# Issuing the zero fill of y_rows from Pool in three parts during the attention, in a fused attention, expert and MLP kernel

## The chip, the cores and the metric

The kernel runs on one core of a Trainium2 chip. The metric is device time in microseconds (us) of one launch, taken over repeated executions; lower is better. The core has a matrix engine (PE), a vector engine (DVE), a scalar engine (ACT), a general engine (Pool, also called GpSimd) and a sync engine (SP) that does little but issue DMAs. Engines run side by side, each through its own list of instructions in order, and meet at semaphores. Data moves between HBM and on-chip SBUF on 16 DMA engines. A DMA that SP issues goes into one hardware queue ("q1 hardware_dynamic" in the profile), one that Pool issues into a software queue ("q0 software_dynamic"); both are served by the same 16 engines.

## The reference

Three stages run one after the other. Attention: 4 batches, 8 heads, 576 positions, head size 64; four heads see a causal band of 32 positions, the other four see every 32nd position. Its output is x, 2304 token rows of 512. Experts: a token whose skip score is above zero goes to the one of 8 experts that its gate picks; its row becomes x plus a gated expert output, all others keep x. MLP: 512 to 2048, leaky ReLU, back to 512.

```python
x = np.ascontiguousarray(attn_out.transpose(0, 2, 1, 3)).reshape(B * S, H * D)
# experts
do_compute = x @ w_skip > 0
xc = x[do_compute]
e_idx = np.argmax(xc @ w_gate, axis=1)
for e in range(E):
    mask = e_idx == e
    h = np.maximum(xc[mask] @ w1[e], 0.0)
    y[mask] = gate_w[mask, None] * (h @ w2[e])
out[do_compute] = xc + y
# MLP
h = x @ w_in
return np.maximum(0.01 * h, h) @ w_out
```

## The kernel before

**Attention.** Each batch has 11 groups of queries (`NG`): 6 of the local heads, 5 of the strided ones. PE transposes q and k in 16 chunks per batch, computes scores, transposes the probabilities and multiplies by v; ACT copies chunks and takes exponentials; DVE subtracts maxima and normalises into `xo`. A loop runs over batches 0 to 2 with the next batch's chunks woven in, and the last batch follows. SP feeds it by hand-written order (`batch`, L449): after each group's `xo` it stores rows to the HBM tensor `x_rows` (`x_store`, L386), loads v of the next batch (`v_load`: L396 for a local group, four DMAs on L401 for a strided one) and, at groups 2, 4, 6 and 8, half of q or k of the batch after that into `q_st` and `k_st` (L409). These staging tiles are copied into `q_in` and `k_in` by three engines. Pool has three of these copies in each of its three loop turns (L616 to L624), in the order q half 0, k half 0, k half 1; each waits for PE to be done with the old chunks and for the load. ACT does q half 1 (L842).

**Routing.** When a batch's `x_rows` have landed, SP loads them back token by token (`x_load`, L441 to L447). PE computes the gate scores, DVE turns them by a long chain of small steps into a list of token numbers per tile of 160 rows (`tok_idx`), and Pool gathers the rows of tile 0 in two halves (`gather_x(0)`, L667), which PE transposes (L1480) before the first expert matmul (L1497).

**Experts.** Tiles 0 to 21 at most; 7 are certain to hold rows written in any case. SP keeps the weights of the next tile coming in a ring of 8 pieces (`half_load`, L360) and stores each tile's result to the HBM tensor `y_rows` (L493, L495). While tiles run, Pool gathers the next tile's rows, loads and splits the MLP weights (`stage_load`, L684), and sorts.

**MLP.** Pool gathers x and y rows in sorted order (L744), PE does the two matmuls in six steps, and results are scattered out. It takes the last 415 us, PE nearly always busy.

**The zero fill.** The gather of `y_rows` in the MLP also reads rows that no tile has written: slots past an expert's last token, and the one row `SKIP` (3520) for tokens that are passed on. Rows 1120 to 3519, `(E - 1) * TILE` to `SKIP`, and row 3520 are therefore set to zero from `zrow`, a tile of zeros in SBUF that Pool sets in its set-up (L596). SP issues both DMAs once, after the last `x_load` and ring pieces 4 to 7 of tile 0 (L480, L481). The big one moves 2400 rows of 2 KB: `zrow` has `FILL` = 120 partitions, each written out `ZC` = 20 times. SP waits for both (L520) before its first tile step, since from then on tiles may store into the same rows, and again at its end (L550); Pool waits for them (L766) before the MLP's first gathers.

Of the kernel before, what the change touches and what calls it, by code (L numbers as in the profile page):

```python
# [17 lines left out]
TILE = 160  # L18
# [4 lines left out]
def attention_experts_mlp(nc, q, k, v, w_skip, w_gate, w1, w2, w_in, w_out, out):  # L23
    B, H, S, DH = q.shape
    E, D, F = w1.shape
# [16 lines left out]
    for r0 in R0:  # L42
        n = min(RES, STRIDE - r0)
# [7 lines left out]
    SKIP = TILES * TILE  # L51
# [9 lines left out]
    y_d = nc.dram_tensor("y_rows", [SKIP + 1, D], F32).ap()  # L61
# [10 lines left out]
    def at(cursor, name, shape, dt=F32):  # L72
        n = size[dt]
        for d in shape[1:]:
            n *= d
        t = nc.alloc_sbuf_tensor_at(name, shape, dt, offset=cursor[0])
        cursor[0] += (n + 31) // 32 * 32
        return t
# [14 lines left out]
    gate3 = at(keep, "gate3", [P, MT])  # L93
    wg = at(keep, "wg", [P, KD, E + 1])
    wgs = at(keep, "wgs", [P, KD, 2 * (E + 1)], F32R)
    ZC = 20
    FILL = (SKIP - (E - 1) * TILE) // ZC
    zrow = at(keep, "zrow", [FILL, D])
    ring0 = keep[0]
# [5 lines left out]
    q_in = at(a, "q_in", [TP, 8, H * DH])  # L105
# [99 lines left out]
    with ExitStack() as ctx:  # L205
# [3 lines left out]
        def sem(name):  # L209
            return ctx.enter_context(nc.semaphore(name))  # L210
# [3 lines left out]
        s_vz = sem("s_vz")  # L214
        s_wg = sem("s_wg")
        s_zd = sem("s_zd")

        s_qs = [sem("s_qs0"), sem("s_qs1")]
        s_ks = [sem("s_ks0"), sem("s_ks1")]
# [193 lines left out]
        def heads_in(dst, src, hs):  # L413

            w_ = slice(HL * DH * hs, HL * DH * (hs + 1))
            return (dst[:, :, w_].rearrange("p c (h d) -> p c h d", h=HL),
                    src[:, HL * hs:HL * hs + HL, :].rearrange("p h (c d) -> p c h d", c=8))
# [3 lines left out]
        def _(sp):  # L421
# [55 lines left out]
            for n in range(4, 2 * NU):  # L477
                half_load(sp, 0, n)

            sp.dma_start(y_d[SKIP:SKIP + 1, :], zrow[0:1, :]).then_inc(s_zd, 16)  # L480
            sp.dma_start(y_d[(E - 1) * TILE:SKIP, :].rearrange("(p c) n -> p c n", p=FILL),  # L481
                         zrow[:, :].unsqueeze(1).to_broadcast([FILL, ZC, D])).then_inc(s_zd, 16)

            sp.wait_ge(s_plan, 2)
            tiles = sp.value_load(plan[0:1, 31:32], min_val=E, max_val=TILES)
# [12 lines left out]
            def tile(i0, d):  # L498
                nxt = i0 + (d + 1)

                def half_done(n):

                    k_ = i0 * FC + (d * FC + 2 * (n // 2) + 2)
                    sp.wait_ge(s_l2 if n % 2 else s_l1, k_)

                def y_before():
                    if not (isinstance(i0, int) and d == 0):
                        y_store(i0 + (d - 1))

                with sp.If(nxt < tiles):  # L510
                    ex_ = sp.value_load(plan[0:1, bass.ds(nxt, 1)], min_val=0, max_val=E - 1)
                    for n in (0, 2, 1, 4, 3, 6, 5, 7):
                        if n == 1:
                            y_before()
                        half_done(n)
                        half_load(sp, ex_, n)
                with sp.Else():
                    y_before()

            sp.wait_ge(s_zd, 32)  # L520
            tile(0, 0)
            with sp.Fori(0, E // 2 - 1) as i2:
                for u in range(2):
# [23 lines left out]
                sp.dma_start(out_tok[:, HEAD + j, :], o_sb[:, j, :]).then_inc(s_oh, 16)  # L547
            sp.wait_ge(s_out, 16 * MT * (NM - 1))
            sp.wait_ge(s_oh, 16 * MT)
            sp.wait_ge(s_zd, 32)  # L550
            sp.wait_ge(s_sct, 16 * NT)


# [1 line left out]
        def _(pool):  # L555
# [48 lines left out]
            def carry():  # L604

                pool.sem_inc(s_tick, 1)
# [6 lines left out]

            with pool.Fori(0, B - 1) as b:  # L616
                for hs, dst, src, s_load, s_in in ((0, q_in, q_st, s_qs[0], s_qi[0]),
                                                   (0, k_in, k_st, s_ks[0], s_ki[0]),
                                                   (1, k_in, k_st, s_ks[1], s_ki[1])):
                    pool.wait_ge(s_tq, len(CH) * b + 8 * (hs + 1))  # L620
                    pool.wait_ge(s_load, 16 * b + 32)
                    carry()
                    to, what = heads_in(dst, src, hs)
                    pool.tensor_copy(to, what).then_inc(s_in, 1)  # L624

# [108 lines left out]
            def indices(m):  # L736
                pool.tensor_copy(idx3[:, 0, :], column(m * MT, 0)).then_inc(s_i3, 1)
                pool.tensor_copy(idx3[:, 1, :], column(m * MT, 1)).then_inc(s_i3, 1)
                pool.wait_ge(s_i3, m * 2 + 2)
                carry()  # L740
# [22 lines left out]
                        bounds_check=N - 1, oob_is_err=False).then_inc(s_out, 16)  # L763

            pool.wait_ge(s_srt, 16)
            pool.wait_ge(s_zd, 32)  # L766
            indices(0)
            gather_rows(x3, x_flat, 0, N - 1, s_gm)
            need = pool.value_load(plan[0:1, 29:30], min_val=1, max_val=TILES)
# [890 lines left out]
```

## Time and profile before

| | us |
|---|---|
| median of 3 runs | 772.04 (771.41 to 774.05) |
| the profiled execution, whole | 777.4 |
| its span in the trace | 775.2 |
| PE busy | 716.9 (92% of the span) |
| DVE busy | 276.2 (36%) |
| ACT busy | 262.0 (34%) |
| Pool busy | 180.5 (23%) |

The trace is of one execution, 5.4 us above the median. Issue of DMAs is not counted as busy time, so SP has no busy row; its work shows as "SPq" in the chain. The chain is the series of steps, each released by the one before it, that ends with the last instruction; its time adds up to the span. "DMA share" is the mean busy share of the 16 DMA engines; it can read a little above 1. The granted clock of PE is 1.00 at 2.4 GHz and 0.50 at 1.2 GHz. Over time the kernel falls into attention (0 to about 157 us), routing (to 202), experts (to 360) and MLP (to the end).

### The profile page before, as it was taken

Reading aid. Unit: us, or ns where it says so; the run is one execution under the profiler, and the core shown is the slowest. Engines: PE = TensorE matmul, PEld = TensorE weight load, DVE = VectorE, ACT = ScalarE, POOL = GpSimd, SP = SyncE. Lnnn points to the kernel's source line nnn. Section 1 sums busy time; section 2 is a strip of 40 time slices with the busy share of each in tenths; the row PEclk is TensorE's granted clock in tenths of the full one; section 3 lists DMA queues with packets and bytes.
Section 4 is the critical chain, followed back from the end, with each engine's and each line's share of the span. In section 5 each row is a group of like instructions: output and inputs, shape, how many; then the busy total and the mean of one; then the engine's idle time right before and its main releaser. Section 6 shows DMA issues by size and latency. Waiting matters only on the chain.

```text
span 775.2 us, 12846 instructions
## 1 busy us (share of the span) xinstructions
PE 716.9 (92%) x4628; PEld 664.1 (86%) x4628; DVE 276.2 (36%) x578; ACT 262.0 (34%) x522; POOL 180.5 (23%) x182
## 2 busy tenths in 40 slices
PE   2989979993699999998999999999999999999997
PEld 2878868873699999997999999998989899999986
DVE  4667656757100000003332333233333333332222
ACT  4687666651111112212222223322232322222222
POOL 2120100011686666562100310040031004001000
PEclk9999998986699999999999999999999999999999
DMA  8483746779799999972100210030012004001001
GB/s 175 107 188 100 168 102 171 218 236 229 168 317 341 300 314 338 315 248 64 43 1 0 70 54 1 7 116 1 1 59 63 0 0 122 0 0 41 1 0 41
DMA packets 73112, 91.46 MB, mean 118 GB/s; under 512 B 26704, under 2 KB 47728, under 8 KB 73073
## 3 DMA queue, kind: packets, MB, share of 16 engines
q1 hardware_dynamic: 63969, 66.14, 29.7%
q0 software_dynamic: 8048, 24.79, 11.3%
q8 instruction: 24, 0.39, 0.2%
q10 hardware_dynamic: 1056, 0.02, 0.1%
q14 instruction: 15, 0.12, 0.0%
HBM read 73.91 MB, written 17.01 MB: 117 GB/s over the span
## 4 chain that ended last, share of the span: by engine, by line
PE 74%; SPq 10%; DMA 5%; DVE 3%; issue 3%; ACT 2%; another core or an unknown queue 2%; ACTq 0%; DVEq 0%; POOLq 0%
PE psum L1584 26%; PE psum L1603 26%; PE psum L1497 8%; PE psum L1513 8%; SPq L401 6%; DMA x_rows<-xo 3%; SPq L396 2%; SPq L386 1%; ACT kt L797 1%; PE psum L1336 1%; PE psum L1523 1%; PE psum L1566 1%; DMA x_sb<-x_rows 1%; SPq L409 1%
## 5 line engine op out<-in xcount | busy, mean ns | idle before, releaser
L1584 PE MATMUL psum<-x2h,wih 128*128 128x384 f32 x384 | 130.6, 340 | 1.9 <-DVE x2l L1256 1.9
L1274 DVE SCALAR_TENSOR_TENSOR g_act<-g_raw 128x384 f32<-128x384 f32 x96 | 53.6, 558 | 219.4 <-ACT g_raw L960 205.9
L1584 PE MATMUL psum<-x2h,wil 128*128 128x384 f32 x384 | 129.5, 337 | 0.0
L1584 PE MATMUL psum<-x2l,wih 128*128 128x384 f32 x384 | 129.0, 336 | 0.0
L960 ACT ACTIVATE g_raw<-psum 128x384 f32<-128x384 f32 x96 | 47.2, 492 | 235.3 <-PE psum L1584 232.0
L1603 PE MATMUL psum<-woh,g_l 128*128 128x512 f32 x288 | 114.0, 396 | 0.0
L1603 PE MATMUL psum<-wol,g_h 128*128 128x512 f32 x288 | 113.7, 395 | 0.0
L1603 PE MATMUL psum<-woh,g_h 128*128 128x512 f32 x288 | 112.1, 389 | 0.7 <-DVE g_l L1278 0.7
L1497 PE MATMUL psum<-xt,wring 128*128 128x160 f32 x512 | 80.9, 305 | 0.6 <-issue 0.6
L759 POOL DMA_INDIRECT out_dram<-o_sb,idxo x15 | 15.9, 1061 | 277.8 <-ACT o_sb L955 274.8
L1513 PE MATMUL psum<-hp,wring 128*128 128x160 f32 x512 | 77.6, 299 | 0.0
L1584 PEld LDWEIGHTS psum<-x2h,wih 128*128 128x128 f32 x384 | 72.2, 188 | 5.7 <-DVE x2l L1256 2.1
L1584 PEld LDWEIGHTS psum<-x2l,wih 128*128 128x128 f32 x384 | 72.1, 188 | 3.5
L1497 PEld LDWEIGHTS psum<-xt,wring 128*128 128x128 f32 x512 | 74.0, 194 | 0.8 <-ACT xt L886 0.8
L1278 DVE TENSOR_TENSOR g_l<-g_act,g_h 128x384 fp32r<-128x384 f32 x96 | 53.6, 558 | 56.9 <-ACT g_h L965 55.7
L1513 PEld LDWEIGHTS psum<-hp,wring 128*128 128x128 f32 x512 | 72.2, 190 | 0.2 <-ACT hp L906 0.2
L1584 PEld LDWEIGHTS psum<-x2h,wil 128*128 128x128 f32 x384 | 72.0, 188 | 0.0
L965 ACT ACTIVATE g_h<-g_act 128x384 fp32r<-128x384 f32 x96 | 50.3, 524 | 60.1 <-DVE g_act L1274 57.6
L1603 PEld LDWEIGHTS psum<-woh,g_l 128*128 128x128 f32 x288 | 54.0, 187 | 11.5
L1603 PEld LDWEIGHTS psum<-woh,g_h 128*128 128x128 f32 x288 | 54.1, 188 | 10.0 <-issue 0.7
L1603 PEld LDWEIGHTS psum<-wol,g_h 128*128 128x128 f32 x288 | 54.0, 187 | 9.1
L906 ACT ACTIVATE hp<-psum 128x160 f32<-128x160 f32 x64 | 19.2, 304 | 100.5 <-PE psum L1497 97.1
(177 smaller groups left out, 899.2 us busy)
## 6 DMA issues: line engine op xcount, KB each, us to landing
wring<-in_moe_w_dram SPq DMA_DIRECT2D x64, 512.0 KB, 8.6
y_rows<-zrow SPq DMA_DIRECT2D x1, 4800.0 KB
q_st<-in_q_dram SPq DMA_DIRECT2D x8, 576.0 KB
k_st<-in_k_dram SPq DMA_DIRECT2D x8, 576.0 KB
x_sb<-x_rows SPq DMA_DIRECT2D x4, 1024.0 KB, 6.4
stage<-in_moe_w_in_dram POOLq DMA_DIRECT2D x4, 1024.0 KB, 9.0
stage<-in_moe_w_out_dram POOLq DMA_DIRECT2D x4, 1024.0 KB, 9.2
vs<-in_v_dram SPq DMA_DIRECT2D x20, 128.0 KB, 7.6
```

Of the source, the lines that this page charges most:

```text
L396: eng.dma_start(vs[lo:P, g, :, 0:DH], src).then_inc(s_v[g], 16)
L401: eng.dma_start(vs[0:G["m"], g, h, 0:DH], src).then_inc(s_v[g], 16)
L759: pool.indirect_dma_start(out=out, out_offset=bass.IndirectOffsetOnAxis(ap=idxo[:, j:j + 1].bitcast(U32), axis=0), in_=o_sb[:, j, :], in_o ...
L906: act.activation(hp[:, f % 4, :], bank[f % 2][:, 0:TILE], ACT.Relu).then_inc(s_hp, 1)
L960: act.activation(g_raw[:, f % 2, :], bank[f % 2][:, 0:MT * P], ACT.Copy).then_inc(s_mr, 1)
L965: act.activation(g_h[:, f % 2, :], g_act[:, f % 2, :], ACT.Copy).then_inc(s_mh, 1)
L1274: dve.scalar_tensor_tensor(out=g_act[:, f % 2, :], in0=g_raw[:, f % 2, :], scalar=LEAK, in1=g_raw[:, f % 2, :], op0=ALU.mult, op1=ALU.max) ...
L1278: dve.tensor_tensor(g_l[:, f % 2, :], g_act[:, f % 2, :], g_h[:, f % 2, :].bitcast(F32), ALU.subtract).then_inc(s_ml, 1)
L1497: last = pe.matmul(bank[f % 2][:, 0:TILE], wring[:, 2 * u_, w_], xt[:, T.par, c, :], start=(c == 0), stop=(c == KD - 1))
L1513: last = pe.matmul(Y[:, c, 0:TILE], wring[:, 2 * u_ + 1, w_], hp[:, f % 4, :], start=(f == 0), stop=(f == FC - 1))
L1584: last = pe.matmul(bank[f % 2][:, 0:MT * P], wt[:, c, f * P:(f + 1) * P], xp[:, T.par, c, :], start=(c == 0 and n == 0), stop=(c == KD - 1 ...
L1603: last = pe.matmul(bank[4 + j][:, :], gt[:, f % 2, j * P:(j + 1) * P], wt[:, f // 4, w_], start=(f == 0 and n == 0), stop=(f == FC2 - 1 an ...
```

## The change

The fill of rows 1120 to 3519 is taken from SP's list. Pool issues it instead as three DMAs of 800 rows each, one in each turn of its attention loop, right behind its copy into `q_in`. `ZC` goes from 20 to 24, so that three parts of 8 rows per partition come out even; `FILL` falls with it from 120 to 100 partitions. The parts count on a semaphore of their own, `s_zf`, for which SP and Pool wait beside `s_zd`, which now covers row 3520 alone (still SP's, in its old place).

```diff
-    ZC = 20
+    ZC = 24
     FILL = (SKIP - (E - 1) * TILE) // ZC
...
             sp.dma_start(y_d[SKIP:SKIP + 1, :], zrow[0:1, :]).then_inc(s_zd, 16)
-            sp.dma_start(y_d[(E - 1) * TILE:SKIP, :].rearrange("(p c) n -> p c n", p=FILL),
-                         zrow[:, :].unsqueeze(1).to_broadcast([FILL, ZC, D])).then_inc(s_zd, 16)
...
-            sp.wait_ge(s_zd, 32)
+            sp.wait_ge(s_zd, 16)
+            sp.wait_ge(s_zf, 16 * (B - 1))
             tile(0, 0)
...
+            def zero_rows(b):
+                c0 = b * (ZC // (B - 1))
+                part = y_d[(E - 1) * TILE:SKIP, :].rearrange("(p c) n -> p c n", p=FILL)
+                part = (part[:, c0:c0 + ZC // (B - 1), :] if isinstance(b, int)
+                        else part[:, bass.ds(c0, ZC // (B - 1)), :])
+                pool.dma_start(part, zrow[:, :].unsqueeze(1).to_broadcast(
+                    [FILL, ZC // (B - 1), D])).then_inc(s_zf, 16)
+
             with pool.Fori(0, B - 1) as b:
...
                     pool.tensor_copy(to, what).then_inc(s_in, 1)
+                    if dst is q_in:
+                        zero_rows(b)
```

The same pair of waits takes the place of `wait_ge(s_zd, 32)` at SP's end and ahead of Pool's first MLP gathers.

## Rows read from the trace of the kernel before

**Rows 1.** Chain of waits, whole span: start us, length us, what it is.

```profile
34.58 5.66 DMA q_st<-in_q_dram
...
104.37 5.95 DMA x_rows<-xo
...
194.62 5.33 DMA xg<-x_rows,tok_idx
...
202.03 5.38 PE psum L1497 x24
```

**Rows 2.** Chain of waits, 0 to 145 us, grouped by line; pieces as in Rows 1.

```profile
by line: SPq L401 31.3%; SPq L396 12.1%; issue 10.7%; SPq L386 6.6%; ACT kt L797 6.5%; PE psum L1336 4.4%; SPq L409 4.2%; DMA x_rows<-xo 4.1%; DMA q_st<-in_q_dram 3.9%; PE psum L1361 3.6%; PE psum L1348 1.8%; PE psum L1314 1.5%; DVE sc L101
...
116.82 1.70 PE psum L1336 x8
...
127.72 0.88 PE psum L1336 x8
```

**Rows 3.** Table by stretch: engines' busy us, then granted clock, DMA share, GB/s.

```profile
24.00:34.00 10.00, 9.89 (x94) 9.44 (x94) 7.88 (x17) 6.25 (x12) 2.66 (x2) 1.00 0.30 59
34.00:52.00 18.00, 15.31 (x156) 14.32 (x154) 10.81 (x29) 15.27 (x26) 3.78 (x2) 1.00 0.85 189
52.00:64.00 12.00, 11.06 (x117) 10.68 (x116) 9.65 (x24) 7.80 (x16) 1.89 (x1) 1.00 0.52 138
64.00:68.00 4.00, 3.75 (x41) 3.55 (x39) 3.52 (x11) 3.95 (x9) 0.00 (x0) 1.00 0.27 40
...
78.00:90.00 12.00, 10.94 (x96) 10.34 (x97) 6.52 (x17) 10.30 (x18) 1.89 (x1) 0.86 0.88 187
90.00:104.00 14.00, 13.17 (x137) 12.69 (x135) 11.38 (x28) 8.69 (x17) 1.89 (x1) 1.00 0.43 110
...
156.00:178.00 22.00, 21.23 (x158) 17.71 (x158) 12.54 (x21) 12.20 (x26) 2.35 (x14) 0.87 0.77 248
178.00:200.00 22.00, 4.20 (x45) 3.43 (x43) 15.29 (x54) 1.95 (x4) 5.86 (x5) 0.59 0.88 198
```

**Rows 4.** Timeline of SP: start us, us, line, DMA, count.

```profile
51.59 3.75 SPq L401 DMA_DIRECT2D vs<-in_v_dram  x4
...
87.21 5.62 SPq L401 DMA_DIRECT2D vs<-in_v_dram  x4
...
94.87 3.71 SPq L401 DMA_DIRECT2D vs<-in_v_dram  x4
...
167.33 0.97 SPq L481 DMA_DIRECT2D y_rows<-zrow  x1
...
206.53 23.32 SPq L360 DMA_DIRECT2D wring<-in_moe_w_dram  x10
```

**Rows 5.** Timeline of Pool: start us, us, line, operation, shapes, idle time before it.

```profile
25.97 1.89 POOL L624 COPY k_in<-k_st 72x2048 f32<-72x2048 f32 x1 [1.20 <-DMA k_st<-in_k_dram]
...
54.08 1.89 POOL L624 COPY k_in<-k_st 72x2048 f32<-72x2048 f32 x1 [2.29 <-DMA k_st<-in_k_dram]
...
93.21 1.89 POOL L624 COPY k_in<-k_st 72x2048 f32<-72x2048 f32 x1 [3.69 <-DMA k_st<-in_k_dram]
...
196.12 0.97 POOL L667 DMA_INDIRECT xg<-x_rows,tok_idx  x1 [0.30 <-issue]
197.10 0.86 POOL L684 DMA_DIRECT2D stage<-in_moe_w_in_dram  x1
```

**Rows 6.** Waits of SP, 190 to 210 us: waiting line, releaser, us, times, longest.

```profile
SPq L485 <- DVE plan L1181: 26.7, 1, 26.7
...
SPq L511 <- DMA y_rows<-zrow: 1.1, 1, 1.1
```

**Rows 7.** Timeline of PE from 199.9 and from 200.7 us, columns as in Rows 5.

```profile
199.99 0.80 PE L1480 MATMUL psum<-ident,xg 80*128 80x80 f32 x4 [6.98 <-DMA xg<-x_rows,tok_idx]
...
200.44 0.96 PE L1480 MATMUL psum<-ident,xg 80*128 80x80 f32 x5
```

**Rows 8.** DMAs of `y_rows`, MLP gathers among them: issue to landing, us.

```profile
DMA to landing us min/median/max: 3.7/3.9/4.6
```

More of the change, by code:

```diff
@@ L216, in attention_experts_mlp @@
         s_zd = sem("s_zd")
+        s_zf = sem("s_zf")
         s_qs = [sem("s_qs0"), sem("s_qs1")]
@@ L549, in _ @@
             sp.wait_ge(s_oh, 16 * MT)
-            sp.wait_ge(s_zd, 32)
+            sp.wait_ge(s_zd, 16)
+            sp.wait_ge(s_zf, 16 * (B - 1))
             sp.wait_ge(s_sct, 16 * NT)
@@ L765, in _ @@
             pool.wait_ge(s_srt, 16)
-            pool.wait_ge(s_zd, 32)
+            pool.wait_ge(s_zd, 16)
+            pool.wait_ge(s_zf, 16 * (B - 1))
             indices(0)
```

## The prediction

> **What bounds the kernel now.** I read the chain of waits first, because a moved DMA can only matter where the chain runs through DMA landings, through SP's issuing, or through a wait on the fill. It does so in two stretches: the attention and the joint between routing and experts. From 202 us on the chain is PE work with hardly a gap, and the change touches nothing there.
>
> In the joint, the chain runs through DVE's routing steps and then through Pool's first gather, issued at 194.62 and 5.33 long, to the first expert matmuls [rows 1]. The fill is issued at 167.33 [rows 4], behind four ring pieces, and the DMA engines then show a share of 0.88 at 198 GB/s from 178 to 200 us, when nothing else large is in flight [rows 3]. SP waits 26.7 us for DVE's plan and then only 1.1 us for the fill [rows 6]; its next DMA, the ring piece at 206.53 [rows 4], waits for PE anyway. So the fill holds nobody by its semaphore. It only shares the DMA engines with the first gather.
>
> In the attention the picture is the opposite. SP's issuing of v loads, q and k loads and stores makes up more than half of the chain [rows 2], and two landings stand in it outright: q half 1 of batch 1, issued at 34.58, and an `x_rows` store at 104.37 [rows 1]. Between these, the DMA engines are not full: shares of 0.30, 0.52 and 0.43, but 0.85 and 0.88 in the two busy stretches [rows 3]. When they are full, SP itself gets slower: four L401 loads take 3.75 and 3.71 us at 51.59 and 94.87, and 5.62 us at 87.21, right behind the stretch with a share of 0.88 [rows 3, 4].
>
> **What is removed.** From SP goes one issue of 0.97 us [rows 4]; it then waits 26.7 us for DVE [rows 6], so this is worth nothing. From the DMA engines go 2400 rows of 2 KB, 4.9 MB, between about 168 and 200 us. What gets earlier is the gather. Its second half is issued at 196.12 [rows 5]; the gathers of y rows in the MLP, of the same form and with less beside them, land 3.7 to 4.6 us after issue, 3.9 in the median [rows 8], which would be 200.0. PE begins the first half's four transposes at 199.99, and the second four are under way only after about 200.8, when the engine is at its lower clock: the eight end at 201.4 [rows 7]. The first half would be in by 198.5 and transposed, so the end comes 0.6 us after the second half's landing, at 200.6, and the first matmul about 0.8 us earlier. The bounds are 0, if the second gather takes 4.6 us, and 1.0 at 3.7 us. I take -0.8.
>
> **What is added on Pool.** Three issues. Pool's load of 1024 KB takes 0.86 us to issue and SP's whole fill took 0.97 [rows 4, 5]; a part of 1600 KB lies between 0.86 and, in proportion to its size, 1.3 us. Each one is in front of the wait for k half 0. Pool has been idle there for 1.20, 2.29 and 3.69 us, waiting for that load [rows 5]. So at most 0.1 us of the first shows, on an engine whose copies are not in the chain [rows 2]. Without that cover it would be 3.9 us of Pool time, still ahead of copies with slack. Taken as 0. The third part is issued near 90.5 us, 104 us ahead of the gathers on Pool's own queue.
>
> **Waits.** The waits on `s_zf` have the whole of routing behind them: the last part must have landed by about 110 us, and SP first asks after 195, Pool after 339. Behind SP's wait stands the ring piece of 206.53 [rows 4]. Worth 0 both ways. The memset of fewer partitions and row 3520 in its old place: 0.
>
> **What is added on the DMA engines.** This is the cost. A part is 1.64 MB; at the fill's own 198 GB/s it takes 8.3 us with a share of 0.88 [rows 3], that is 7.3 us of all 16 engines.
>
> Part 0 starts near 25.8 us. Until 34 the engines are idle for 0.70 of 8.2 us = 5.7 us [rows 3], so 1.6 us of it is left when the q load of 34.58 is issued, whose landing is in the chain at full length [rows 1]. I add these 1.6 us. Bounds: 0, if the idle 0.70 is all used and the two share well; 5.7 if the landing doubles.
>
> Part 1 starts near 52.8. To 64 us the engines are idle for 0.48 of 11.2 = 5.4 us, and the remaining 1.9 fit into the 2.9 idle us of 64 to 68 [rows 3]. No landing of the chain lies there; what can suffer is SP's issuing. Of L401 groups two more are issued while the part runs. If each goes from 3.7 to 5.6 us, as at 87.21, that is 3.8 us; if SP's queue stays short it is 0. The group of 51.59 kept 3.75 us right behind a stretch of 0.85, so I take 0.5.
>
> Part 2 starts near 90.5, just as SP is coming out of its slow stretch. To 104 the engines are idle for 0.57 of 13.5 = 7.7 us [rows 3], so it ends just ahead of the store of 104.37. The queue that had slowed SP now drains at about half the rate. I take 1.5 us, between 0 and the 3.8 of two slow groups, nearer to the row of 87.21 than for part 1.
>
> **Sum.** -0.8 + 1.6 + 0.5 + 1.5 = +2.8 us, with ends at -1.0 and +13.3 that would need all to go one way. In the trace's terms: whole time 777.4 to 780.2, span 775.2 to 778.0. The median of the runs is 5.4 us below the profiled execution, and nothing here scales with that, so I put the same 2.8 us on it: 772.04 + 2.8 = 774.8.
>
> **A rule weighed.** While the fill ran, the share stayed at 0.88 where loads in the ring's stretches exceed 1.0, as if one of the engines had no part in it; before, the fill has 120 partitions. The Trainium skill (DMA: Bandwidth & Descriptors, section "Why a DMA increments its semaphore by 16 and not by 1") says that a transfer is spread over the largest number of engines up to 16 that divides its slowest dimension, 15 for 120 and 10 for 100, but that some direct copies issued from Pool are spread over 15 with 100 partitions. The first row agrees with 15; no row here shows 100. What ten engines would do is the narrow rival.
>
> **The rivals.**
>
> Absorbed (same time). The idle share swallows all three parts: both queues are served in turn, the q load of 34.58 finds its engines nearly free, and SP, which was not slowed by shares up to 0.52, is not slowed by short stretches near 1. For it: idle time of 5.7, 8.3 and 7.7 us against 7.3 us of need each [rows 3]. Against it: the first does not fit before 34.58, and the averages hide peaks. It decides as soon as part 0 has landed by about 35 us. Price: -0.8 to +0.5, about 771.5.
>
> Narrow (much slower). The parts run on ten engines instead of 15. Then a part takes 8.3 * 15 / 10 = 12.4 us on them, with about 11.6 us of busy time each; from 25.8 to 34.6 they are idle for 6.1, so 5.5 us are left in front of the q load instead of 1.6. With the other terms as they are: 5.5 + 0.5 + 1.5 - 0.8 = +6.7, or 778.7.
>
> Clock (faster). PE runs at the lower clock around 116 us, after the wait behind the store of 104.37: eight L1336 matmuls take 1.70 us there and 0.88 at full clock [rows 2]. If the moved work shifts that store or PE's pause so that the clock stays up, about 2.4 us come back over that stretch (the rows of the chain from 115.7 to 120.9 at half their length), on top of the 0.8: 768.8. Nothing in the change aims at it, and as easily a further pause is added.
>
> Held issue (slower). Pool's issue of a part takes far longer than 1.3 us, because 800 rows meet a queue that is full, and its k copy comes late. It would have to be late by more than the slack of that copy; then each turn of the loop pays. About 780.
>
> **How the numbers follow.** Forecast (sharing costs 1 to 5 us) 0.38; absorbed 0.34; narrow 0.14; clock 0.11; held issue 0.03. The predicted time is the likeliest case's, 774.8, its own range 772.2 to 776.5. The range of 8 in 10 leaves out most of the clock case below and the tails of narrow and held above: 770.6 to 780.0. About 0.3% (2.3 us) is what a measurement of this kernel can tell from no change, so the line between same and slower is at 774.35. A quarter of the forecast's cases lie below it (0.09), with most of absorbed (0.32): same 0.41. Faster: clock and a little of absorbed, 0.13. Slower: 0.29 + 0.14 + 0.03 = 0.46.
>
> **What the profile would show.** Right, if after the change: the DMA share of 180 to 194 us falls to near 0 and the second gather is landed at about 200.0 with the transposes in one piece; the q load of 34.58 lands after more than 6.5 us; the last `xo` comes 3 to 4 us later than before. Absorbed, if that load still takes 5.7 us and SP's L401 groups 3.7. Narrow, if a stretch with nothing but the fill shows a share near 0.6. Held, if Pool's issue lines are longer than 1.3 us. The prediction is wrong in its main step if the end of the attention does not move, and in its sign if the gather turns out to have been held by the fill by much more than 0.8 us, or if PE keeps its full clock through 112 to 121 us.

## The result and the profile after

The changed kernel takes 793.14 us (median of 4 runs, 792.73 to 795.51) against 771.81 for the kernel before beside it: a ratio of 1.0277, with a 95% interval of 1.0248 to 1.0305. That is 21 us slower. The forecast was +2.8 us, with a range up to 780.0: the direction was right, the size was not. In the traces the span goes from 775.2 to 791.3 us.

Lines of the changed kernel stand one below those of before in SP's part: L402 is the strided v load (L401 before), L387 the store, L410 the q and k loads, L397 the local v load. The first view is Pool's timeline, first of before and then of after, at the first step that waits for the whole attention (`c_pref`, released by the last `xo`):

```profile
156.58 0.14 POOL L640 IOTA c_pref<- 128x8 f32 x1 [44.94 <-DVE xo L1034]
```

```profile
24.16 1.28 POOL L622 DMA_DIRECT2D y_rows<-zrow  x1
...
173.11 0.14 POOL L651 IOTA c_pref<- 128x8 f32 x1 [45.40 <-DVE xo L1046]
```

The attention ends 16.5 us later, 173.1 against 156.6. That is the whole loss of the span. Four other runs of this study have the attention of the kernel before, untouched, and end it at 152.7 to 153.8 us, so the profiled execution of before was itself some 3 us slow in the attention (its rows at 84.89 and 87.21, the group of 5.62 us among them, are 2.5 us longer than in the run with the late fill), and against those the change costs it 20 us, as the medians say.

Where in the attention, the chain of waits of after shows (start, us, what), answering to [rows 1, 2]:

```profile
25.48 0.75 SPq L402
...
26.27 2.20 SPq L402
...
28.51 1.77 SPq L402
...
30.32 2.11 SPq L402
...
32.48 1.91 SPq L402
...
34.42 0.75 SPq L402
...
38.73 5.95 DMA q_st<-in_q_dram
```

The kernel before at the same place (its chain):

```profile
22.11 1.94 SPq L401
24.09 1.41 SPq L401
25.55 0.75 SPq L401
26.34 0.75 SPq L401
27.13 0.75 SPq L401
```

Right behind Pool's issue of part 0, four of SP's loads take 2 us each instead of 0.75. (Two loads near 22 and 24 us take 1.2 to 2.0 us in the other profiles too, before included, with no part of the fill in flight; why was not looked into.) The q load that I had expected to suffer lands after 5.95 us, against 5.66 [rows 1], only it is issued at 38.73 instead of 34.58. The other two parts show in SP's timeline, answering to [rows 4]:

```profile
57.63 6.07 SPq L402 DMA_DIRECT2D vs<-in_v_dram  x4
63.90 1.42 SPq L410 DMA_DIRECT2D q_st<-in_q_dram  x1
...
101.04 3.26 SPq L410 DMA_DIRECT2D q_st<-in_q_dram  x1
104.56 1.28 SPq L387 DMA_DIRECT2D x_rows<-xo  x1
106.05 8.01 SPq L402 DMA_DIRECT2D vs<-in_v_dram  x4
```

Part 1 is issued at 57.95 and part 2 at 99.27. Added up against the same instructions of before, SP's issue rows are 4.5 us longer behind part 0 (20 loads on L402 in 21.92 us instead of 17.39), 4.6 behind part 1 and about 8 behind part 2. Since SP's issuing is in the chain there, these rows make up the loss. Beside the run with the late fill (below), whose attention is untouched and ends at 152.7 us, they are 5.0, 4.6 and 8.4 us longer, 18.1 of its 20.4 us. The same instruction of SP comes 5.2 us later there behind part 0, 10.9 behind part 1 and 19.6 behind part 2.

The DMA share behind part 0 (columns as in [rows 3]), and the time from issue to landing of the parts:

```profile
26.00:30.00 4.00, 4.00 (x31) 3.80 (x30) 2.60 (x5) 1.94 (x4) 1.35 (x1) 1.00 0.70 199
30.00:34.00 4.00, 4.00 (x47) 3.94 (x46) 3.23 (x7) 3.18 (x7) 0.00 (x0) 1.00 0.61 202
```

```profile
DMA to landing us min/median/max: 12.3/12.7/16.7
```

So SP is held while about a third of the DMA engines' time is unused (a quarter beside parts 1 and 2: shares of 0.71 from 58.5 to 70 us and 0.77 from 100 to 111.5). A part takes 12.7 us, not 8.3.

The gain at the joint came too (chain of after):

```profile
210.77 1.10 POOL xg L678
212.16 2.96 DMA xg<-x_rows,tok_idx
...
216.59 6.53 PE psum L1509 x24
```

From the gather's issue to the first expert matmul it is 5.8 us instead of 7.4 [rows 1], 1.6 us less. (The lines show the gather's second half; both halves are counted.) Of this the first 24 matmuls give back 1.15, at 6.53 against 5.38 us: they run longer at the lower clock.

### The profile page after: what moved, and what is told of

Its sections match the earlier page's. It is cut to its first block, busy times and chain, and to the rows that moved or that the text cites. A ratio compares the mean times of both kernels' runs of the same rounds, so it can differ in the third digit from the quotient of the medians.

```text
span 791.3 us, 12857 instructions
## 1 busy us (share of the span) xinstructions
PE 727.6 (92%) x4628; PEld 675.3 (85%) x4628; DVE 275.7 (35%) x578; ACT 263.2 (33%) x522; POOL 183.9 (23%) x185
## 4 chain that ended last, share of the span: by engine, by line
PE 78%; SPq 12%; DVE 3%; DMA 3%; issue 2%; ACT 2%; POOL 0%; ACTq 0%; DVEq 0%; POOLq 0%
PE psum L1596 26%; PE psum L1615 25%; PE psum L1509 9%; PE psum L1525 9%; SPq L402 7%; SPq L397 2%; DMA x_rows<-xo 2%; SPq L387 1%; PE psum L1348 1%; SPq L410 1%; PE psum L1446 1%; PE psum L1463 1%; PE psum L1373 1%; PE psum L1535 1%; PE psum L1578 1%
## 5 line engine op out<-in xcount | busy, mean ns | idle before, releaser
L1290 DVE TENSOR_TENSOR g_l<-g_act,g_h 128x384 fp32r<-128x384 f32 x96 | 53.6, 558 | 57.1 <-ACT g_h L977 54.7
## 6 DMA issues: line engine op xcount, KB each, us to landing
y_rows<-zrow POOLq DMA_DIRECT2D x3, 1600.0 KB, 12.7
```

Source lines behind the costliest of these rows:

```text
L1290: dve.tensor_tensor(g_l[:, f % 2, :], g_act[:, f % 2, :], g_h[:, f % 2, :].bitcast(F32), ALU.subtract).then_inc(s_ml, 1)
```

## The experiments

All times are medians beside runs of the kernel before on the same chip (772.9 to 774.2 us). "Attention end" is the start of `c_pref` in the profiled execution.

**One part alone, the shape, and the old place.** First, only part 0 stays with Pool:

```diff
-                    if dst is q_in:
+                    if dst is q_in and turn == 0:
```

> Pool issues only the first of the three parts (800 rows, first loop turn); SP issues the other 1600 rows once the plan is there. In the changed kernel the attention ends 16.5 us later than before (173.1 against 156.6), and SP's own issue rows account for 4.6, 4.6 and 8.4 us behind parts 0, 1 and 2. Alternation theory (while a part is in flight each small descriptor of a v load waits for one 2 KB descriptor of the fill on the same engine, and SP's issue waits with it): the parts add up one by one, the attention ends 4 to 5 us later than before, about 161, and only the L402 loads issued between 26 and 37 us are long. Fullness rival (SP slows down because the 16 engines together are full): about the same number, but the long loads would be those of 38 to 48 us, where the share is 0.9. Clock rival (most of the loss is PE at its lower clock after added pauses): the first part alone costs 8 us or more, since it already makes such a pause.

Attention end 160.2; the L402 loads behind the part take 2.16, 1.68, 2.13 and 2.05 us, and all groups of four from 57.88 us on are at 3.7 again (one of 4.07 at 92.67 aside). So the part brings its loss at once, and the long loads are those of 26 to 35 us. The fullness rival is out. Against the untouched attentions the one part costs 6.3 to 7.4 us, of which the twenty loads have 5.3 (22.19 us against 16.90 in the run with the late fill). PE's lower clock is then a small share of it, and the clock rival, which asked for 8 us or more, fails too, though by little. The total, 789.9 us (1.0193, 1.0147 to 1.0239), is higher than this for another reason, which the run with the late fill shows. Then the shape alone:

```diff
-    ZC = 24
+    ZC = 30
```

> The changed kernel with 80 partitions of 30 rows instead of 100 of 24: the same bytes and the same 2 KB rows in the same three issues, but the slowest dimension is 80, which 16 divides. Alternation: 50 fill rows per engine and part instead of 80, so SP's extra issue time falls to 50/80 of 17.6 us, some 11 us; a part lands after about 8 us instead of 12.7; total 6 to 7 us below the changed kernel, 786 to 787. Width rival (the ten engines are the whole cause, the idle share would take the parts if they were spread): total within 3 us of the kernel before, about 774. If the number of engines has nothing to do with it: 793.

Measured 783.9 us (1.0139, 1.0102 to 1.0177), attention end 165.6, a part 9.2 to 10.0 us to landing. Half of the loss is gone, somewhat more than alternation said and far less than width alone. While the part is there a load takes the same 2 us:

```profile
27.12 2.08 SPq L402
...
29.24 2.29 SPq L402
```

What shrinks is the time in which loads are slow. The same question was put to the old place, the kernel before with `ZC` = 24:

> The kernel before with nothing changed but the shape of the fill, 100 partitions of 24 rows on SP's queue in its old place. If 100 partitions put it on ten engines and 120 on fifteen, it takes about 33 us instead of 22, the DMA share falls from 0.88 to about 0.6 while it runs alone, SP gets past its wait only near 211 us and the ring pieces of 206.5 come some 5 us late. Attention end unchanged, 156.6. Width theory: total +0 to +3 us against before. If the width is the same: total unchanged within 1 us and the share stays 0.88.

Measured 777.5 us (1.0056, 1.0036 to 1.0077), just slower. While the fill ran alone the share was 0.63 instead of 0.90, as expected, though the GB/s stayed at 205. SP waited 8.5 us for it instead of 1.1, but the loss is not SP's: it is the first gather, issued at 191.00, which lands only 10.0 us later, against 5.3 [rows 1]: the first expert matmul comes 12.0 us after its issue instead of 7.4. So the change of `ZC` by itself was worth 4 us there.

**The fill after the plan.** To see what the removal alone is worth, SP issues all of it behind the first gather:

```diff
             sp.wait_ge(s_plan, 2)
+            sp.dma_start(y_d[(E - 1) * TILE:SKIP, :]...)
...
-            sp.wait_ge(s_zd, 32)
             tile(0, 0)
...
+            sp.wait_ge(s_zd, 32)
             tile(0, E - 1)
```

> No fill in the attention and none before the first gather: SP issues the whole fill (120 partitions) only when the plan is there, behind Pool's first gather, and waits for it ahead of the step of tile 7, the first whose rows it shares. This measures what the removal alone is worth. My step (the fill delays the first gather by 0.8 us): 0.5 to 1.0 us below before, 771.0. The changed kernel's rows say more: from the gather's issue to the first expert matmul 5.8 us against 7.4, so -1.6 us, 770.2. Rival (the fill now collides with the second tile's gathers and the weight loads of 200 to 220 us): 0 to +3 us.

Measured 786.5 us (1.0179, 1.0141 to 1.0217), worse than any of the expectations. The fill now delays two gathers, that of tile 0 and that of tile 1 (the second half of each, chain of that kernel):

```profile
191.75 10.56 DMA xg<-x_rows,tok_idx
...
205.62 12.03 DMA xg<-x_rows,idx
```

Without a fill beside it such a gather lands in 3.0 us, as in the changed kernel. The first expert matmul comes 13.5 us after the first gather's issue, where it is 6.0 in the run of 96 partitions below, and the block of 24 matmuls of line L1513 behind tile 1's gathers starts 24.0 us after that instead of 17.8. Together this is 13.7 us, and the spans of these two runs differ by 13.0. So the fill does to Pool's gathers of 80 rows what it does to SP's v loads, the other way round: the small transfer of one queue is held up beside the large one of the other. The two runs that leave part of their fill this late (one_part above, tiny below) pay the same.

**What in the fill slows SP down.** My theory was turn-taking by descriptor, that is by single pieces of the two transfers. It makes the size of the pieces decisive:

```diff
-                pool.dma_start(part, zrow[:, :].unsqueeze(1).to_broadcast(
-                    [FILL, ZC // (B - 1), D])).then_inc(s_zf, 16)
+                part = part.rearrange("p c (s n) -> p (c s) n", n=P)
+                pool.dma_start(part, zrow[:, 0:P].unsqueeze(1).to_broadcast(
+                    [FILL, ZC // (B - 1) * (D // P), P])).then_inc(s_zf, 16)
```

> The changed kernel with each 2 KB row of the fill written as four runs of 512 bytes: same bytes, same engines, same moments, four times the descriptors. In the changed kernel four L402 loads in a row take 2.20, 1.77, 2.11 and 1.91 us beside part 0 instead of 0.75. Alternation theory (one descriptor of the v load, one of the fill, in turn; 18 v descriptors per engine times some 0.12 us for a 2 KB one): a 512-byte descriptor holds the v load for a third or less, so an L402 load beside the fill takes 0.8 to 1.2 us; the fill itself lasts longer, and the total falls by 5 to 12 us against the changed kernel, to 781 to 788. Rival, time shares (each queue gets its part of an engine's time, whatever the size of its pieces): L402 stays at 2 us for as long as the fill runs, and the total stays at 793 or rises.

```diff
+                pool.dma_start(part.rearrange("p c n -> p (c n)"),
+                               wring[0:FILL, 4:8, :].rearrange("p a n -> p (a n)")).then_inc(s_zf, 16)
```

> The changed kernel with each part written as 100 runs of 16 KB from a zeroed piece of the weight ring instead of 800 runs of 2 KB (the four late ring pieces wait for the fill to land, which it has long before). Same bytes, engines and moments, an eighth of the descriptors. Alternation by descriptor: 18 v descriptors each wait for a 16 KB one, so SP stands still until the fill is through; a part costs up to its whole length of 12 us, total 800 or more. Alternation by a fixed unit of bytes (the engine cuts long runs): as the changed kernel, 793. Rival, rates: fewer descriptors make the part quick, 8 us or less instead of 12.7, and the loss falls by a third, 786.

With pieces of 512 bytes 800.0 us (1.0338, 1.0291 to 1.0386), with 16 KB 781.3 us (1.0107, 1.0070 to 1.0145). My theory is refuted: it had the order the wrong way round. Five loads beside the small pieces take 2.17, 1.89, 1.81, 2.11 and 1.78 us, three beside the large ones 1.85, 1.61 and 1.41. The length of a slow load is much the same for pieces of 512 bytes and 2 KB and a little less for 16 KB. What the size changes most is how long a part is there:

| rows of the fill | a part, issue to landing, us | attention end | ratio |
|---|---|---|---|
| 16 KB pieces, 100 partitions | 8.0 | 161.7 | 1.0107 |
| 2 KB, 80 partitions | 9.7 | 165.6 | 1.0139 |
| 2 KB, 100 partitions (the change) | 12.7 | 173.1 | 1.0277 |
| 512 bytes, 100 partitions | 19.9 | 183.4 | 1.0338 |

**Whether it is Pool.** Same issues with an eighth of the bytes, and the same parts from another engine:

```diff
+                part = part[:, bass.ds(b, 1), :]
+                pool.dma_start(part, zrow[:, :].unsqueeze(1)).then_inc(s_zf, 16)
```

> Pool issues three parts at the changed kernel's moments, but of one row per partition (100 rows, 200 KB each instead of 1600); SP issues the other 2100 rows once the plan is there. This keeps Pool's issues and takes away seven eighths of the bytes. Alternation: each part holds SP for an eighth as long, under 1 us, so the attention ends within 2 us of the kernel before (152.7 to 156.6 in four profiles of that attention). Rival, generator (Pool's making of descriptors or its shared port disturbs SP's issue, whatever the size): the attention still ends 10 us or more later. The total is 786 to 788 in either case for the late rest, by the run that issues all rows late.

```diff
             def rest(b, last):
                 for s_ in range(2, NG):
+                    if s_ == 3 and not last:
+                        zero_rows(b)
```

> The same three parts (100 partitions, 8 rows of 2 KB) issued by ACT instead of Pool, at about the same moment of each batch (before its work on group 3), through ACT's hardware queue. Alternation on the DMA engines does not care who issues: SP's L402 loads beside a part take 2 us again, the attention ends 15 to 20 us later than before, and the total is 790 to 796, with 1 us more per part if ACT's issue is in the way. Rival, software queue (it is Pool's descriptors that slow SP's): L402 stays at 0.75, and the total comes down to 775 to 779.

Tiny parts: attention end 154.1, L402 at 0.75 right behind the issue; total 787.0 (1.0172, 1.0130 to 1.0215), which is the late rest. Pool's issuing of so small a part costs nothing that shows. Issued by ACT through its hardware queue: 794.9 us (1.0269, 1.0225 to 1.0312), attention end 175.1, and the loads beside the part (issued at 30.0) are slow again:

```profile
31.14 2.17 SPq L402
...
33.36 1.42 SPq L402
...
34.82 1.75 SPq L402
...
36.62 1.39 SPq L402
```

The q load behind them lands after 8.1 us, so here the landing suffers too. So it takes neither Pool's queue nor Pool's issue to slow SP down. It is the transfer.

**The moment.** The parts behind Pool's third copy of the turn:

```diff
-                    if dst is q_in:
+                    if hs:
```

> The changed kernel with each part issued behind Pool's third copy of the turn (k half 1, near 45, 75 and 113 us) instead of the first (near 25, 53, 91). Lasting theory: what a part costs is the number of SP's strided v loads (L402) that fall into its 12 us, if SP is then in the chain. Part 0 now falls where SP issues q, k and local v loads and waits for the stores' results, part 1 into the last strided loads and the refill, part 2 into the stretch behind 113 us in which PE, ACT and DVE set the pace. So the loss shrinks: attention end 160 to 167, total 780 to 787. Rival (a part costs the same wherever it is put): 173, total 793.

Measured 791.8 us (1.0229, 1.0197 to 1.0261), attention end 173.5: no better. My expectation named the strided loads alone, but the other instructions of SP are held as well (timeline of SP; part 0 is issued at 45.11 and part 1 at 79.76):

```profile
51.96 8.88 SPq L402 DMA_DIRECT2D vs<-in_v_dram  x4
...
82.62 3.58 SPq L397 DMA_DIRECT2D vs<-in_v_dram  x2
86.45 1.99 SPq L387 DMA_DIRECT2D x_rows<-xo  x1
```

The L397 pair of before takes 0.99 us at that place. SP has something small to issue everywhere in the attention, and the later moment in the turn lost as much. The first two parts meet fuller stretches here than in the change (before has a share of 0.76 from 44 to 58 us and 0.85 from 78 to 92), and SP falls 5.7 and 6.8 us behind in them, about what the parts of the change cost (4.6 to 8.4): how idle the 16 engines are on average does not set the price.

**Which engines.** Fewer engines for longer:

```diff
-    ZC = 24
+    ZC = 96
```

> The changed kernel with 25 partitions of 96 rows: same bytes, same 2 KB rows, same three issues, but few engines carry them (the slowest dimension is 25, so 5). So far an L402 load beside the fill takes 1.4 to 2.3 us instead of 0.75, whatever the size of the fill's pieces, and the attention ends the later the longer the parts last (a part of 8.0, 9.7, 12.7, 19.9 us to landing: 161.7, 165.6, 173.1, 183.4 us). Lasting theory (SP's small loads are slow for as long as the fill is present on any engine they use, and how full the 16 engines are does not matter): a part lasts 20 to 26 us and the attention ends at 183 or later, total 800 or more, although the 16 engines' share is only raised by a third at a time. Rival, load on the engines: most of a v load's engines have no fill on them, so the L402 loads are shorter than 2 us and the total is no worse than the changed kernel's, 793.

Measured 793.6 us (1.0269, 1.0238 to 1.0300), attention end 175.1: neither theory's number. The parts differ among themselves. Pool's issues, then SP's loads:

```profile
61.76 1.32 POOL L622 DMA_DIRECT2D y_rows<-zrow  x1
...
108.30 1.28 POOL L622 DMA_DIRECT2D y_rows<-zrow  x1
```

```profile
69.26 10.91 SPq L402 DMA_DIRECT2D vs<-in_v_dram  x4
...
113.13 3.69 SPq L402 DMA_DIRECT2D vs<-in_v_dram  x4
...
118.12 3.69 SPq L402 DMA_DIRECT2D vs<-in_v_dram  x4
```

Parts 0 and 1 hold SP for longer than in the change; behind part 2, in flight for some 20 us, SP's strided loads keep their 3.69 us. Presence alone is therefore not enough. Here the Trainium skill helps (DMA: Bandwidth & Descriptors, section "Why a DMA increments its semaphore by 16 and not by 1"): a transfer of fewer than 16 engines takes the lowest-numbered ones if SP issues it, and the next ones in turn if Pool does. A strided v load has a slowest dimension of 7, so it would be on engines 0 to 6, and the three parts of 25 partitions on 0 to 4, 5 to 9 and 10 to 14, if Pool's turn starts at 0. No row names the engines, but the third part fits. Two runs put it to the test: the same six DMAs, 20 rows on ten engines and 780 rows on six in each turn, in two orders.

```diff
+                pool.dma_start(few[bass.ds(b, 1)]..., zrow[0:10, :] ... [10, 2, D])
+                pool.dma_start(part[bass.ds(b, 1)]..., zrow[0:6, :] ... [6, 130, D])
```

> The changed kernel with each part split in two DMAs: first 20 rows from 10 partitions, then 780 rows from 6 partitions (130 rows each). If Pool's DMAs of fewer than 16 engines take the engines in turn, one DMA behind the other, the small one uses engines 0 to 9 and the large one 10 to 15, in every turn of the loop. Overlap theory: SP's issue of a strided v load (126 rows, 7 of them slowest, so the first 7 engines) is slow only while the fill is on one of its own engines, as the third part of the run with 25 partitions suggests, beside which L402 groups kept 3.69 us. Then L402 stays at 3.7 us for all three parts, although each lasts 20 us or more, the attention ends at 153 to 158, and the total is 770 to 775. Rival, presence (any transfer in flight slows SP, and the third part was an accident of the place): attention end 173 or later, total 790 or more.

> The same six DMAs as in the run with the large ones on the high engines, in the other order: the large one first (engines 0 to 5, if they are taken in turn), then the small one (6 to 15). Same bytes, same number of engines, same moments. Overlap theory: all three parts now lie on the v loads' engines for 20 us or more: L402 groups beside them take 8 us and more, as in parts 0 and 1 of the run with 25 partitions, the attention ends at 180 or later, total 795 or more. Rival, number of engines and time in flight alone: equal to the other order within 2 us.

Timeline of SP, the small one first:

```profile
16.51 17.23 SPq L402 DMA_DIRECT2D vs<-in_v_dram  x20
...
50.03 21.01 SPq L397 DMA_DIRECT2D vs<-in_v_dram  x1
...
86.18 4.19 SPq L402 DMA_DIRECT2D vs<-in_v_dram  x4
...
148.02 3.69 SPq L402 DMA_DIRECT2D vs<-in_v_dram  x4
```

and the large one first:

```profile
17.44 54.66 SPq L402 DMA_DIRECT2D vs<-in_v_dram  x20
...
105.66 30.48 SPq L402 DMA_DIRECT2D vs<-in_v_dram  x4
...
174.26 32.47 SPq L402 DMA_DIRECT2D vs<-in_v_dram  x4
```

The large parts are issued at 24.44, 83.26 and 144.96 us in the first run and at 24.86, 90.74 and 163.12 in the second. The order alone decides over the strided loads, in all three turns: 17.2 us for twenty, as in the kernel before, against 54.7, then 4.2 and 3.7 us for a group against 30.5 and 32.5. Two DMAs of ten and six engines fill one round of 16, so by the rule the order changes which engines the large one is on and little else. No row names them, but two arrangements (25 partitions, and these) came out as the overlap of engines says, and the presence rival fails on the strided loads. The totals, 853.9 us (1.1055, 1.1027 to 1.1083) and 885.9 (1.1447, 1.1421 to 1.1474), missed my first number by far (770 to 775), and its attention ends at 235.0 us: six partitions feed a fill at a crawl, up to 53.5 us to landing, and the loads that are spread wider, q, k and the local v (21.0 us for one), then stand behind it in either order.

**Two trials at a better old place.**

```diff
-    ZC = 20
+    ZC = 25
```

> The kernel before with the fill's shape alone changed, to 96 partitions of 25 rows, in SP's old place: a slowest dimension of 96 is spread over all 16 engines instead of 15 (the run with 100 partitions and 10 engines cost 0.6%). The fill ends about 1.4 us earlier, the first gather lands 0.5 to 1 us earlier, total 0 to 1 us below before. If the width plays no part there: no change.

```diff
-            x_load(B - 1)
             for n in range(4, 2 * NU):
                 half_load(sp, 0, n)
+            x_load(B - 1)
```

> The kernel before with SP's ring pieces 4 to 7 issued ahead of the last load of x_rows instead of behind it, so that they use the DMA engines' gap (158 to 164 us, share 0.46 to 0.04) and the fill runs from about 167 to 190, ahead of the first gather at 194.6. If the gather is what the fill costs in its old place: 1.5 to 2 us below before. Rival: the pieces slow down the last stores of x_rows, whose landing (156.63 to 163.5) is in the chain, by more than the gather gains: 0 to +4 us.

Rows of 96 partitions: 0.9993 (0.9975 to 1.0011); ring pieces first: 1.0007 (0.9984 to 1.0030). Neither differs measurably from the kernel before. In the profile the first did what it should (chain):

```profile
191.15 3.03 DMA xg<-x_rows,tok_idx
...
195.64 6.51 PE psum L1497 x24
```

```profile
175.00:185.00 10.00, 1.51 (x20) 1.32 (x20) 8.87 (x33) 0.95 (x2) 1.30 (x1) 0.64 0.90 305
```

The fill moves 305 GB/s over this stretch, 350 up to 182 us where it ends soon after, instead of 203, and is gone before the gather, which lands at the undisturbed 3.0 us; the 24 matmuls take 6.51 us instead of 5.38. The second run has the gather's 2.9 us without the longer matmuls (5.19), and loses on the last load of `x_rows` (8.46 us, where the chain of before has 6.51). By these rows neither can be worth more than about 1 us, and the medians cannot tell that from nothing.

## Why the prediction was wrong

**What bounds the kernel.** Right: SP's issuing is the chain in the attention, and the fill in its old place holds only the first gather. The gain of 0.8 us was 1.6, above the bound of 1.0, for the free landing is 3.0 us where I took 3.9 from gathers of another stage. Two thirds of it went back to the clock.

**Pool's issues and the waits.** Right. Issue rows of 1.02 to 1.28 us lie in the estimated 0.86 to 1.3; the k copies move by nothing that shows, and no wait on `s_zf` is in the waits.

**The cost on the DMA engines: the step that failed.** I worked out each part as 7.3 us of all 16 engines against their idle time, and let it be absorbed where the mean share was low. Part 0 was to cost 1.6 us, all of it in the landing of the q load. It cost 0.3 there and 4.5 before it, in SP's issue, at a share of 0.6 to 0.7. Part 1 was put at 0.5 and took 4.6, part 2 at 1.5 and took about 8. In its place the runs showed that SP's issue of a small load is held for as long as a part is in flight on the load's own engines: the loss grows with how long a part lasts (8.0 to 19.9 us), not with the mean share, and it goes for the strided loads when the order of two DMAs puts the part on other engines. The mean over 16 engines says nothing of the few that a small transfer uses. How an engine divides its time between the two queues, and why SP's issue has to wait for it, no run shows.

**The bounds.** The row from which I took the upper end pointed the right way: a group of 5.6 us instead of 3.7 [rows 4], though it was a slow one of that execution (4.0 us at the same place with the late fill). I read it as the effect of a full set of engines, so I allowed it for two groups per part and for none in part 0. Beside a part a group takes up to 8.0 us, and part 0 meets four loads of the set-up that the sum did not price at all.

**The narrow rival.** Its premise held: 12.7 us per part against the 12.4 worked out, and a share of 0.61. Its price, +6.7, was still made with idle time, and too small by three times. With 80 partitions, which the rule weighed in the prediction puts on 16 engines, the change is still 1.4% slower, so the ten engines are half of the loss, not its cause.

**The absorbed and the clock rival.** Nothing was absorbed. The granted clock of PE is at or near 0.50 in two stretches of the attention before (86 to 90 and 114 to 120 us) and in four after (46 to 52, 86 to 92, 118 to 124 and 132 to 140), each behind a pause of PE: the longer pauses added such stretches. What this costs was not measured apart, but SP's rows leave no more than 2.3 of the 20.4 us for it and all else.

## What to carry to other kernels

Before a bulk transfer is moved into a "quiet" stretch, do not ask how idle the DMA engines are on average, but which small transfers are in flight there, on how many engines, and whether their issuer is in the chain: beside bulk data on the same engines their issue or landing took two to four times as long here, until the bulk was through. If it must go there, keep it short (here 80 partitions lost half as much as 100, and pieces of 16 KB less than half of what pieces of 2 KB lost); the old place, behind everything else, was better than any moment tried in the attention. And a factor changed only to make parts come out even, here 120 partitions to 100, is a change of its own that wants its own run.

## What the runs showed of the hardware that was not expected

- An SP load of 126 short rows takes 0.75 us to issue, and 1.4 to 2.3 us while another queue has bulk data in flight: 1.8 to 2.3 beside Pool's pieces of 512 bytes and 2 KB, 1.4 to 1.9 beside its 16 KB, 1.4 to 2.2 beside ACT's 2 KB.
- A Pool gather of 80 rows lands in 3.0 us alone and in 10.0 to 12.0 us beside SP's fill.
- 4.9 MB of zeros went out at 203 GB/s from 120 partitions (share 0.90, 180 to 192 us), 205 GB/s from 100 (share 0.63, 178 to 190 us) and 350 GB/s from 96 (share 1.03, 176 to 182 us). Why 120 is no faster than 100 is open.
- A part of 1.6 MB from 6 partitions took up to 53.5 us; one from 100 partitions took 12.7.
